# Linear attention's second pass: pairs of products joined to 104 columns, another order of products, and the prefix scan first

## The chip, the cores and the metric

The kernel runs on one NeuronCore of a Trainium2 chip. The metric is the time of one execution on the device in microseconds; the median of three runs is taken. The engines are named PE (TensorE), DVE (VectorE), ACT (ScalarE), POOL (GpSimd) and SP (the engine that only issues transfers here). All arithmetic that the change touches is in 32-bit floating point.

## The reference

Three stages follow each other. The change touches only the first, a linear attention with a state of 40 x 40 per head (4 batches, 8 heads, 768 positions):

```python
for t in range(S):
    y[:, :, t] = np.einsum('bhd,bhde->bhe', rt, state)
    Sa = np.einsum('bhde,bhe->bhd', state, at)
    state_decay = state * wt[:, :, None, :] - np.einsum('bhd,bhe->bhde', Sa, bt)
    state = state_decay + np.einsum('bhd,bhe->bhde', vt, kt)
```

The second stage routes each of 3,072 tokens to one of 8 experts by the largest of 8 logits (a product with `moe_w_gate`), two products with a ReLU between, weighted by the gate. The third is a dense layer with a leaky ReLU (320 to 2,048 to 320).

## The kernel before

Attention is done in chunks of 64 positions. There are 24 steps (`STEPS`): 12 chunks for each of two halves of the batch. A step handles 16 heads at once: two partition halves (rows 0 to 39 and 64 to 103 are live) times eight slots (`HS`). Every product of a step is 16 matmuls (`heads`: four slots times `COMBOS`, the four 64 x 64 quadrants of the array). The trace shows a 32-bit matmul as two records, so a group of 16 matmuls is 32 records and 32 weight loads.

The first pass (to 131 us) makes, per step, scans of the decay w over the chunk on DVE, products for the chunk's triangular system, and its inverse in blocks (POOL does most of the inverting, until about 294 us, beside the second pass). The scans are two: suffix products (`suffixes`, backward, into `suf`) and prefix products (`prefixes`, forward, into `wq`), the second started from the reciprocal of the first's end (`prefix_starts`).

The second pass (139 to 375 us) carries the state through the steps. PE runs one loop (`pe.Fori`, L930) with 18 groups, in this order by the names of the operands: alpha with the scaled state `swt` (and with `ax`, alpha brought across the halves by a transfer), values `vtm` with `g2`, the state turned (`eye,swt`), the keys turned (`eye,second`), u (`w_tm,inv`), m1 (`rr,vt`), `vtm,ktm`, the low part (`sa_tm,off`), `eye,st`, `m,ktm`, sa (`w_tm,inv`), sat (`inv,w_tm`), `rr,st`, `sa_tm,btm`, m2 (`rr,sat`), g2 (`alpha,second`), picks (`pick,yt`: rows of x and logits), `m,btm`. `arrive` is a wait on a semaphore. The products go to four pairs of PSUM banks (BA to BD). The new state is the sum of `vtm,ktm`, `eye,st` and `sa_tm,btm` in BD; the output is the sum of `m,ktm`, `rr,st` and `m,btm` in BB.

ACT copies products from PSUM to SBUF (L745 w_tm, L747 st, L749 ktm, L751 and L756 sa_tm, L758 sat, L738 picked) and spreads the inverse into `inv` (L722). DVE scales alpha (L454) and second (L451), masks m1, m2 and g2 (L482), adds the low part to w_tm (L529), scales the state (L548) and the output (L459), sums the gate parts (L464), and makes the scans for the step after next. The order on each engine is the order of the code; SP issues loads in the order of its own loop. After step 24 come the routing (from L561) and the experts.

Of the kernel before, what the change touches and what calls it, by code (L numbers as in the profile page):

```python
# [10 lines left out]
ALU = mybir.AluOpType  # L11
# [4 lines left out]
PARTS = 128  # L16
BATCH, HEADS, SEQ, DIM = 4, 8, 768, 40
HALF = PARTS // 2
C = 64
# [82 lines left out]
WIDE = C + 2  # L102
GROUP = PARTS // (4 * HS)
# [49 lines left out]
BLOCK_AT = B * B + B  # L153
BY_DVE, AT_DVE = 2, 11
# [5 lines left out]
def attention(nc, inp, dram, keep):  # L160

    with ExitStack() as ctx:
# [11 lines left out]
        alpha, second = (m_.sb(n, [PARTS, HS, C]) for n in ("alpha", "second"))  # L174
# [5 lines left out]
        btm, ktm, st = (m_.sb(n, [PARTS, HS, DIM]) for n in ("btm", "ktm", "st"))  # L180
        g2, m1, m2, sat, vt = (m_.sb(n, [PARTS, HS, C]) for n in ("g2", "m1", "m2", "sat", "vt"))
        rr = m_.sb("rr", [PARTS, HS + HP, C])
        vtm = m_.sb("vtm", [PARTS, HS + HP, DIM])
        inv = m_.sb("inv", [PARTS, HS, C])
        inv_in = ring("inv_in", 2, [PARTS, HS, B])
        w_tm, sa_tm, swt = (m_.sb(n, [PARTS, HS, DIM]) for n in ("w_tm", "sa_tm", "swt"))
# [4 lines left out]
        logit = m_.sb("logit", [PARTS, NTT, EXPERTS])  # L191
        ROUTE = NTT * EXPERTS
        late = m_.sb("late", [PARTS, 5 * ROUTE + NET * EXPERTS])

        def late_part(n, **sizes):
# [41 lines left out]
        s_set, s_suf, s_rw, s_wq, s_wc, s_second, s_alpha1, s_alpha0, s_alpha = (m_.sem(n) for n in (  # L237
            "s_set", "s_suf", "s_rw", "s_wq", "s_wc", "s_second", "s_alpha1", "s_alpha0", "s_alpha"))
        names = ("turned", "across", "joint", "g1", "bt", "w", "s", "u", "ktm", "z", "m1", "sa", "sat", "st", "g2", "m2", "y", "pick")
        did = {n: m_.sem("pe_" + n) for n in names}  # L240
        out_of = {n: m_.sem("ev_" + n) for n in names}
        s_settle = m_.sem("s_settle")
        s_xst = [m_.sem(f"s_xst{s}") for s in two]
        s_rows, s_iota = m_.sem("s_rows"), m_.sem("s_iota")
# [25 lines left out]
        def _(sp):  # L270
            def load_t(j):
                if j >= TR:
                    if j - TR < STEPS:
                        sp.wait_ge(s_alpha1, j - TR + 1)
                    elif j - TR == STEPS:
                        sp.wait_ge(s_alpha0, 1)
                    else:
                        sp.wait_ge(s_second, j - TR + 1)
                src = inp["wab"][j] if j < STEPS else inp["wak"][j - STEPS]
                sp.dma_start(t_in[j % TR][:, :], src).then_inc(s_t[j % TR], 16)  # L280
# [41 lines left out]
            def load_rr(k):  # L322
                if k >= 1:
                    sp.wait_ge(did["m2"], k)
                sp.dma_start(rr[:, :, :], inp["rr"][k]).then_inc(s_vt_rr, 16)

            def load_vtm(k):
                if k >= 1:
                    sp.wait_ge(did["z"], k)
                sp.dma_start(vtm[:, :, :], inp["vtm"][k]).then_inc(s_ax_vtm, 16)  # L330

            def load_vt(k):
                if k >= 1:
                    sp.wait_ge(did["m1"], k)
                sp.dma_start(vt[:, :, :], inp["vt"][k]).then_inc(s_vt_rr, 16)

            def cross_wq(k):
                sp.wait_ge(s_wc, k + 1)
                if k >= 3:
# [1255 lines left out]
```

## Time and profile before

| | |
|---|---|
| runs | 1055.56, 1056.46, 1059.53 us (median 1056.46) |
| profiled execution | 1057.93 us, its span 1056.2 us |
| PE, DVE, ACT, POOL busy over the span | 953.4, 710.1, 442.8, 269.8 us |
| first pass | 0 to 131 us, DVE busy 92% of its first 70 us |
| second pass | 139 to 375 us |
| routing and turn to the experts | 375 to 400 us |
| experts, dense layer | 400 to 678 us, 678 to 1056 us |

The span is cut into instructions by engine. "Idle before" is the time in which the engine had nothing running ahead of an instruction. A matmul's record includes the time in which its result drains, so records of one group overlap and the start of the next group tells more than the end of the last. A group's line gives the start of its first record, the time from there to the end of its last, and the number of records.

### The profile page before, as it was taken

To read this page: it belongs to the slowest core of one execution; us is meant where nothing else is said; L and a number is where in the kernel's file an instruction comes from. 1 tells how busy PE (TensorE), PEld (TensorE's weight loads), DVE (VectorE), ACT (ScalarE), POOL (GpSimd) and SP (SyncE) were. 2 spreads that over 40 slices of the span, in tenths; PEclk is the share of its full clock that TensorE was granted. 3 is DMA by queue.
4 is the path that set the end of the run, shared out by engine and by line. 5 is a ranking of instruction groups with operands and counts; after the bars stand their busy time and mean duration, and the time that the engine had idled before them with its cause. 6 is when DMAs were issued, how large, how long until landed. Compare 5 with 4: busy or idle time off the path is not lost. (4 is left out here: it accounts for less than half of the span.)

```text
span 1056.2 us, 48691 instructions
## 1 busy us (share of the span) xinstructions
PE 953.4 (90%) x21425; PEld 875.1 (83%) x21425; DVE 710.1 (67%) x1076; ACT 442.8 (42%) x940; POOL 269.8 (26%) x348
## 2 busy tenths in 40 slices
PE   3426779999999998999999999879999999999997
PEld 2426769999989958898999999668999999999997
DVE  8997947899988764554555555557665565656654
ACT  5525635755556604555555555513222212222211
POOL 1009989798910003213111100240001000000000
PEclk9999977999999999999999999989999999999999
DMA  7968856889888539999676755120100101010100
GB/s 234 256 192 212 216 142 202 254 270 262 259 251 255 171 119 296 310 297 303 192 246 213 228 169 168 42 77 10 39 4 26 25 1 25 2 26 1 25 1 26
DMA packets 118354, 159.62 MB, mean 151 GB/s; under 512 B 68516, under 2 KB 87860, under 8 KB 117908
## 3 DMA queue, kind: packets, MB, share of 16 engines
q1 hardware_dynamic: 103956, 125.12, 39.8%
q0 software_dynamic: 5872, 25.28, 8.0%
q10 hardware_dynamic: 8464, 8.43, 2.4%
q8 instruction: 36, 0.59, 0.2%
q14 instruction: 26, 0.21, 0.1%
HBM read 133.15 MB, written 19.23 MB: 144 GB/s over the span
## 5 line engine op out<-in xcount | busy, mean ns | idle before, releaser
L1466 ACT CAST g_hi<-g 128x512 fp32r<-128x512 f32 x96 | 59.5, 620 | 279.2 <-DVE g L1410 275.5
L1319 PE MATMUL y_bank<-w_out_hi,g_hi 128*128 128x320 f32 x380 | 119.1, 313 | 4.8 <-DVE g_lo L1384 2.9
L1107 PE MATMUL h_bank<-xt,w 128*128 128x128 f32 x992 | 121.4, 280 | 1.0 <-issue 0.8
L1147 DVE TENSOR_TENSOR w_lo<-w_all,w_hi 128x640 fp32r<-128x640 f32 x124 | 101.6, 825 | 29.1 <-ACT w_hi L1187 22.4
L1107 PEld LDWEIGHTS h_bank<-xt,w 128*128 128x128 f32 x992 | 114.5, 193 | 5.8 <-issue 1.9
L1319 PE MATMUL y_bank<-w_out_hi,g_lo 128*128 128x320 f32 x380 | 118.0, 311 | 0.0
L1319 PE MATMUL y_bank<-w_out_lo,g_hi 128*128 128x320 f32 x380 | 117.9, 310 | 0.0
L1406 DVE TENSOR_SCALAR neg<-h_bank,slope 128x512 f32<-128x512 f32 x96 | 71.9, 749 | 66.9 <-PE h_bank L1306 62.8
L1306 PE MATMUL h_bank<-xt_hi,w_in_hi 128*128 128x512 f32 x288 | 113.6, 394 | 0.5 <-DVE xt_hi L1367 0.5
L1306 PE MATMUL h_bank<-xt_hi,w_in_lo 128*128 128x512 f32 x288 | 112.7, 391 | 0.0
L1384 DVE TENSOR_TENSOR g_lo<-g,g_hi 128x512 fp32r<-128x512 f32 x96 | 66.5, 693 | 65.9 <-ACT g_hi L1466 63.8
L1140 DVE SCALAR_TENSOR_TENSOR ht_lo<-h_bank,ht_hi 128x512 fp32r<-128x512 f32 x62 | 42.7, 691 | 91.2 <-ACT ht_hi L1180 90.1
L1187 ACT CAST w_hi<-w_all 128x640 fp32r x124 | 89.8, 727 | 27.2 <-PE y_bank L1119 17.5
L127 POOL TENSOR_TENSOR solved<-solved,share 128x31 f32<-128x31 f32 (+15 forms) x124 | 96.6, 779 | 9.7
L782 PE MATMUL bank<-alpha,second 40*64 40x64 f32 x1568 | 45.2, 271 | 56.6 <-DVE alpha L454 55.8
L124 POOL TENSOR_TENSOR share<-solved,blk 128x31 f32<-128x31 f32 (+15 forms) x124 | 93.2, 752 | 9.7
L782 PEld LDWEIGHTS bank<-alpha,second 40*64 40x64 f32 x1568 | 39.1, 180 | 59.9 <-issue 59.9
L95 POOL DMA_INDIRECT x<-x_rows_mid,order x31 | 31.6, 1019 | 192.9 <-DVE order L607 96.7
L1319 PEld LDWEIGHTS y_bank<-w_out_hi,g_hi 128*128 128x128 f32 x380 | 71.9, 189 | 10.3 <-DVE g_lo L1384 4.0
L1119 PE MATMUL y_bank<-w_hi,ht_hi 128*128 128x320 f32 x248 | 79.1, 319 | 0.0
L1180 ACT ACTIVATE ht_hi<-h_bank 128x512 fp32r<-128x512 f32 x62 | 37.0, 598 | 100.0 <-PE h_bank L1107 95.3
L1119 PE MATMUL y_bank<-w_lo,ht_hi 128*128 128x320 f32 x248 | 76.7, 309 | 0.0
(213 smaller groups left out, 2146.3 us busy)
## 6 DMA issues: line engine op xcount, KB each, us to landing
w<-w_in SPq DMA_DIRECT2D x31, 1024.0 KB
t_in<-wab_in SPq DMA_DIRECT2D x24, 776.0 KB, 4.6
t_in<-wak_in SPq DMA_DIRECT2D x24, 776.0 KB, 6.0
w_all<-w_in POOLq DMA_DIRECT2D x8, 1280.0 KB, 9.4
rr<-rr_in SPq DMA_DIRECT2D x24, 384.0 KB, 3.4
w_rest<-w_in SPq DMA_DIRECT2D x62, 128.0 KB
vt<-vt_in SPq DMA_DIRECT2D x24, 256.0 KB, 3.8
vtm<-vtm_in SPq DMA_DIRECT2D x24, 240.0 KB, 3.4
```

Source lines behind the costliest of these rows:

```text
L124: link(eng.tensor_tensor(part, q[:, 0:j + 1, j:j + 1].to_broadcast(shape), h[:, j:j + 1, j + 1:B].to_broadcast(shape), ALU.mult))
L127: link(eng.tensor_tensor(rest, rest, part, ALU.subtract))
L782: last = pe.matmul(out[HALF * to:HALF * to + rows_out, row, n * i:n * i + n], lhs, rhs, start=opens and i == 0, stop=closes and i == HP - 1)
L1107: last = pe.matmul(h_bank[s][h][:, f * ET:(f + 1) * ET], w1[s][:, k, (FH * h + f) * PARTS:(FH * h + f + 1) * PARTS], xt[s][:, k, :], start ...
L1119: last = pe.matmul(y_bank[s][:, 0:FEAT], h[s][:, f, :], w[:, f, :], start=f == 0 and n == 0, stop=f == NF - 1 and n == 2)
L1147: dve.tensor_tensor(piece(w2_lo, p), of_expert(e, p), piece(w2_hi, p).bitcast(F32), ALU.subtract).then_inc(s_w2lo, 1)
L1187: act.copy(piece(w2_hi, p), of_expert(e, p)).then_inc(s_w2hi, 1)
L1306: last = pe.matmul(h_bank[j % 2][:, :], w[:, k, f * PARTS:(f + 1) * PARTS], x_part[b % 2][:, k, :], start=n == 0, stop=n == len(passes) - 1)
L1319: last = pe.matmul(y_bank[n][:, 0:FEAT], g_part[j % RING][:, n * PARTS:(n + 1) * PARTS], v[:, f, :], start=f == 0 and p == 0, stop=f == NF ...
L1384: dve.tensor_tensor(g_lo[j % RING][:, :], g[j % 2][:, :], g_hi[j % RING][:, :].bitcast(F32), ALU.subtract).then_inc(s_glo, 1)
L1406: dve.tensor_scalar(neg[j % 2][:, :], h_bank[j % 2][:, :], 0.0, keep.slope[:, f:f + 1], ALU.min, ALU.mult).then_inc(s_neg, 1)
L1466: act.copy(g_hi[j % RING][:, :], g[j % 2][:, :]).then_inc(s_ghi, 1)
```

## The change

In the second pass, four pairs of products with one stationary operand each are joined into products of 104 columns (`BOTH`). The moving operands stand side by side in new tiles: `alpha_eye` (alpha beside the identity), `eye_rr` (identity beside r), `v_m1` (values beside m1), `sa_m2` (sa beside m2). The state and the output now stand side by side in bank BD, so both are complete when the last group is. The loop of PE has 14 groups in another order. `vtm,g2` runs first, and alpha with the state waits for its end (`did["gv"]`), and for the scaled state. The keys are turned at the end of the step before, beside g2.

The prefix scan comes first in both passes and its end gives the decay of the chunk; the suffix scan starts from its reciprocal. The copy L448 falls away. The gate parts are copied by ACT (`gate_parts`) and reduced by DVE in two instructions at the end, not in one per step. ACT copies the values into `v_m1`. Loads of `t_in` (from the fourth on), `rr` and `vt` bring 112 partitions (`USED`) and not 128; `vtm` brings 8 slots and not 12. Some tiles lie on space of later stages.

```diff
+BOTH = C + DIM
+USED = HALF + 48
@@ DVE, the second pass
             for k in range(STEPS):
                 more = k + 1 < STEPS
-                if k >= 1:
-                    y_out(k - 1)
-                    if k >= 2:
-                        gates_of(k - 2)
-                    else:
-                        dve.sem_inc(out_of["pick"], 1)
                 dve.wait_ge(did["w"], k + 1)
                 if more:
-                    scaled_alpha(STEPS + k + 1, s_alpha)
+                    scaled_alpha(STEPS + k + 1).then_inc(s_alpha, 1)
                 if k + 2 < STEPS:
-                    suffixes(STEPS + k + 2)
-                dve.wait_ge(did["m1"], k + 1)
-                masked(m1, BB).then_inc(out_of["m1"], 1)
-                if k + 2 < STEPS:
-                    prefix_starts(STEPS + k + 2)
+                    if k >= 1:
+                        dve.wait_ge(out_of["y"], k + 1)
+                    prefixes(STEPS + k + 2)
+                    suffix_starts(STEPS + k + 2)
                 dve.wait_ge(did["z"], k + 1)
                 w_flat = w_tm[:, :, :].rearrange("q (r p) e -> q r (p e)", r=2)
                 dve.tensor_tensor(w_flat, w_flat, BA[:, :, 0:HP * DIM], ALU.add).then_inc(out_of["z"], 1)
+                dve.wait_ge(did["m1"], k + 1)
+                masked(m1, wide(BB)).then_inc(out_of["m1"], 1)
                 if more:
-                    dve.wait_ge(did["ktm"], k + 1)
                     scaled_second(STEPS + k + 1)
                 else:
                     dve.sem_inc(s_second, 1)
                 if k + 2 < STEPS:
-                    prefixes(STEPS + k + 2)
+                    suffixes(STEPS + k + 2)
                 elif k + 2 == STEPS:
                     dve.wait_ge(s_iota, 8)
+                    dve.wait_ge(s_gates, NTT - LATE)
+                    first_choices(gates_of(FIRST))
                     choices_top(FIRST, first_choices)
...
@@ ACT
+            def key_out(k):
+                act.wait_ge(out_of["g2"], k + 1)
+                if k >= 1:
+                    act.wait_ge(did["st"], k)
+                act.copy(by_row(ktm[:, :, :]), BC[:, :, 0:HP * BOTH].rearrange("q r (p t) -> q r p t", t=BOTH)[:, :, :, C:BOTH]).then_inc(out_of["ktm"], 1)
...
+                act.copy(v_m1[:, :, 0:DIM], vtm[:, :, :]).then_inc(s_beside, 1)
...
@@ PE, the loop of the second pass
             with pe.Fori(1, STEPS + 1) as i:
                 arrive(s_ax_vtm, 48 * i)
+                arrive(out_of["g2"], i)
+                heads(g2_v, BA, DIM, closes=False, done="gv")
                 arrive(out_of["st"], i)
-                heads(alpha_s, BA, DIM, closes=False)
-                arrive(out_of["g2"], i)
-                heads(g2_v, BA, DIM, opens=False, done="w")
+                arrive(did["gv"], i)
+                heads(alpha_s, BA, DIM, opens=False, done="w")
+                heads(turned_state, BB, DIM, done="s")
+                arrive(out_of["w"], i)
+                arrive(out_of["ktm"], i)
+                heads(u_product, BC, DIM, done="u")
                 arrive(out_of["y"], i)
...
```

PE, the loop of the second pass, before. A row is an instruction or a run of equal ones; the last numbers are stationary by moving columns, and the tiles are named by what they hold (`m` is m1 or m2).

```order
L782 MATMUL bank<-vtm,g 64x40 [waits ev_g2]
L782 MATMUL bank<-vtm,g 64x40 x15
L782 MATMUL bank<-eye,swt 40x40 [waits ev_y]
L782 MATMUL bank<-eye,swt 40x40 x15
L782 MATMUL bank<-eye,second 64x40 [waits ev_pick]
L782 MATMUL bank<-eye,second 64x40 x15
L782 MATMUL bank<-w_tm,inv 64x40 [waits ev_w]
L782 MATMUL bank<-w_tm,inv 64x40 x15
```

The same place after the change: the tail of alpha with the state, and u behind it.

```order
L793 MATMUL bank<-vtm,g 64x40 [waits s_ax_vtm,ev_g2]
L793 MATMUL bank<-vtm,g 64x40 x15
L793 MATMUL bank<-swt,alpha_eye 64x40 [waits ev_st,pe_gv]
...
L793 MATMUL bank<-eye,swt 40x40 x16
L793 MATMUL bank<-w_tm,inv 64x40 [waits ev_w,ev_ktm]
L793 MATMUL bank<-w_tm,inv 64x40 x15
```

`vtm,g` has moved ahead of the state's products and is waited for; the turned keys no longer stand ahead of u.

PE, the end of the loop, before: from sat to the jump.

```order
L782 MATMUL bank<-inv,w_tm 40x64 x16
L782 MATMUL bank<-rr,st 40x64 x16
L782 MATMUL bank<-sa_tm,btm 40x40 [waits ev_sa]
L782 MATMUL bank<-sa_tm,btm 40x40 x15
L782 MATMUL bank<-rr,sat 64x64 [waits ev_sat]
L782 MATMUL bank<-rr,sat 64x64 x15
L772 REGISTER_ALU
L782 MATMUL bank<-alpha,second 64x64 [waits s_second]
L782 MATMUL bank<-alpha,second 64x64 x15
L772 REGISTER_ALU
L844 MATMUL bank<-pick,yt 64x48 [waits ev_st]
```

The same place after (`w_0` holds sat, `x_1` holds btm, `v_m` and `sa_m` are `v_m1` and `sa_m2`).

```order
L793 MATMUL bank<-eye_rr,st 40x104 [waits s_rows]
L793 MATMUL bank<-eye_rr,st 40x104 x15
L793 MATMUL bank<-eye_rr,w_0 64x64 [waits ev_sat]
L793 MATMUL bank<-eye_rr,w_0 64x64 x15
L782 REGISTER_ALU
L793 MATMUL bank<-alpha_eye,second 64x104 [waits s_second,ev_sa]
L793 MATMUL bank<-alpha_eye,second 64x104 x15
L793 MATMUL bank<-v_m,ktm 40x104 [waits ev_m1,s_beside]
L793 MATMUL bank<-v_m,ktm 40x104 x15
L793 MATMUL bank<-sa_m,x_1 40x104 [waits ev_m2,s_btm]
L793 MATMUL bank<-sa_m,x_1 40x104 x15
```

The product that completes the state was followed by four groups (m2, g2, picks, `m,btm`); now it is the last group of the loop.

DVE, one step of the second pass, before (`TENSOR_TENSOR_SCAN` is printed as SCALAR_TENSOR_TENSOR).

```order
L454 TENSOR_TENSOR alpha<-t_in,wq 128x512 [waits pe_w]
L435 SCALAR_TENSOR_TENSOR suf<-t_in,restart 128x528 [waits s_second,s_t2]
L482 TENSOR_TENSOR m<-bank,later 128x512 [waits pe_m1]
L440 RECIPROCAL restart<-suf 128x8 [waits s_suf]
L529 TENSOR_TENSOR w_tm<-w_tm,bank 128x320 [waits pe_z]
L451 TENSOR_TENSOR second<-t_in,suf 128x512 [waits pe_ktm]
L444 SCALAR_TENSOR_TENSOR wq<-t_in,restart 128x528 [waits s_rw]
L448 COPY wq<-suf 128x8 [waits s_wq]
L548 TENSOR_TENSOR swt<-bank,wq 128x320 [waits s_wqx1,pe_st]
L482 TENSOR_TENSOR m<-bank,later 128x512 [waits pe_m2]
L482 TENSOR_TENSOR g<-bank,later 128x512 [waits pe_g2]
L459 TENSOR_TENSOR yt<-bank,wq 128x512 [waits s_wqx0,pe_y]
```

The same step after.

```order
L469 TENSOR_TENSOR alpha_eye<-t_in,wq 128x8x64 [waits pe_w]
L450 SCALAR_TENSOR_TENSOR wq<-t_in,restart 128x528 [waits s_suf,s_t0,ev_y]
L455 RECIPROCAL restart<-wq 128x8 [waits s_wq]
L530 TENSOR_TENSOR w_tm<-w_tm,bank 128x320 [waits pe_z]
L490 TENSOR_TENSOR v_m<-bank,later 128x8x64 [waits pe_m1]
L466 TENSOR_TENSOR second<-t_in,suf 128x512 [waits s_suf]
L461 SCALAR_TENSOR_TENSOR suf<-t_in,restart 128x528 [waits s_second,s_rw]
L490 TENSOR_TENSOR sa_m<-bank,later 128x8x64 [waits pe_m2]
L490 TENSOR_TENSOR g<-bank,later 128x512 [waits pe_g2]
L557 TENSOR_TENSOR swt<-bank,wq 128x320 [waits s_wqx1,pe_st]
```

The mask of m1 and the add of z have changed places, a whole scan stands ahead of the add, another ahead of the mask of m2, and the scaled state comes after both masks.

## Rows read from the trace of the kernel before

**Rows 1.** Windows of the second pass: start and end, length, busy by engine, clock, DMA.

```profile
138.00:160.00 22.00, 16.40 (x704) 15.74 (x708) 9.32 (x14) 6.93 (x18) 19.14 (x38) 0.67 0.52 147
160.00:370.00 210.00, 201.54 (x12819) 192.46 (x12815) 178.24 (x285) 125.57 (x313) 118.49 (x162) 0.98 0.82 239
```

**Rows 2.** Timeline, one step without GpSimd: start, length, engine, line, operation, tiles.

```profile
329.57 0.22 PE L782 MATMUL bank<-swt,alpha 40*64 40x40 f32 x1 [0.24 <-issue]
330.03 0.68 PE L782 MATMUL bank<-vtm,g 64*64 64x40 f32 x32
330.77 0.43 ACT L745 COPY w_tm<-bank 128x320 f32<-128x320 f32 x1 [1.54 <-PE bank L782]
331.34 0.68 PE L782 MATMUL bank<-w_tm,inv 64*64 64x40 f32 x32
332.84 0.67 PE L782 MATMUL bank<-sa_tm,off 32*64 32x40 f32 x32
333.44 0.52 PE L782 MATMUL bank<-eye,st 40*40 40x40 f32 x32
333.58 0.49 DVE L529 TENSOR_TENSOR w_tm<-w_tm,bank 128x320 f32<-128x320 f32 x1
333.77 0.64 PE L782 MATMUL bank<-m,ktm 64*40 64x64 f32 x32
334.23 0.66 PE L782 MATMUL bank<-w_tm,inv 64*64 64x40 f32 x32
334.67 0.67 PE L782 MATMUL bank<-inv,w_tm 64*40 64x64 f32 x32
335.40 0.59 ACT L758 COPY sat<-bank 128x512 f32<-128x512 f32 x1
336.13 0.69 PE L782 MATMUL bank<-rr,sat 40*64 40x64 f32 x32
336.62 0.68 PE L782 MATMUL bank<-alpha,second 40*64 40x64 f32 x32
336.88 0.69 DVE L482 TENSOR_TENSOR m<-bank,later 128x512 f32<-128x512 f32 x1 [0.24 <-PE bank L782]
337.72 0.66 PE L782 MATMUL bank<-m,btm 64*40 64x64 f32 x32
338.61 0.22 PE L782 MATMUL bank<-swt,alpha 40*64 40x40 f32 x1 [0.23 <-issue]
```

**Rows 3.** Timeline, output scaling of two steps, fourteen steps apart.

```profile
170.68 0.69 DVE L459 TENSOR_TENSOR yt<-bank,wq 128x512 f32<-128x512 f32 x1 [0.21 <-PE bank L782]
300.85 0.69 DVE L459 TENSOR_TENSOR yt<-bank,wq 128x512 f32<-128x512 f32 x1 [0.27 <-PE bank L782]
```

**Rows 4.** Timeline, filler matmuls of 512 columns after the second pass.

```profile
378.82 6.68 PE L849 MATMUL bank<-t_in,ones 128*128 128x512 f32 x15
```

**Rows 5.** Timeline, the scaling of the state at step 22.

```profile
363.63 0.49 DVE L548 TENSOR_TENSOR swt<-bank,wq 128x320 f32<-128x320 f32 x1 [0.34 <-PE bank L782]
```

**Rows 6.** Timeline, PE at the loop's turn while the clock is low.

```profile
155.83 1.10 PE L782 MATMUL bank<-m,btm 64*40 64x64 f32 x32
156.92 0.29 PE L782 MATMUL bank<-swt,alpha 40*64 40x40 f32 x1
```

**Rows 7.** Timeline, reductions on DVE in step 22 and in the routing.

```profile
362.01 0.32 DVE L471 TENSOR_REDUCE top<-logit 128x21 f32<-128x168 f32 x1
377.19 0.18 DVE L471 TENSOR_REDUCE top<-logit 128x3 f32<-128x24 f32 x1
383.17 0.61 DVE L595 TENSOR_REDUCE total<-late 128x24 f32<-128x192 f32 x1
```

**Rows 8.** Timeline, DVE, suffix scans of two steps of the first pass.

```profile
37.69 1.25 DVE L435 TENSOR_TENSOR_SCAN suf<-t_in,restart 128x528 f32<-128x528 f32 x1
41.71 1.25 DVE L435 TENSOR_TENSOR_SCAN suf<-t_in,restart 128x528 f32<-128x528 f32 x1
```

**Rows 9.** Timeline, PE in the first turn of the second pass's loop.

```profile
145.56 0.36 PE L782 MATMUL bank<-vtm,ktm 64*40 64x40 f32 x5 [3.32 <-issue]
```

More of the change, by code:

```diff
@@ L173, in attention @@
         wq = [t[:, 0:HS, :] for t in wq_both]
-        alpha, second = (m_.sb(n, [PARTS, HS, C]) for n in ("alpha", "second"))
+        second = m_.sb("second", [PARTS, HS, C])
+        alpha_eye = m_.sb("alpha_eye", [PARTS, HS, BOTH])
+        alpha = alpha_eye[:, :, 0:C]
         ax = m_.sb("ax", [PARTS, HP, C])
@@ L542, in _ @@
                     choices_one(FIRST, first_choices).then_inc(s_hot, 1)
+                dve.wait_ge(did["m2"], k + 1)
+                masked(m2, wide(BA)).then_inc(out_of["m2"], 1)
+                if more:
+                    dve.wait_ge(did["g2"], k + 2)
+                    masked(g2[:, :, :], beside(BC, 0, C)).then_inc(out_of["g2"], 1)
                 dve.wait_ge(did["st"], k + 1)
+                dve.wait_ge(s_wqx[k % 2], 32 * turn(k))
                 if (k + 1) % NCHUNK == 0:
@@ L742, in _ @@
             prepare(0)
+            key_out(0)
             for k in range(STEPS):
@@ L776, in eye, with heads @@
                 return keep.eye[live(h), HALF * h:HALF * h + DIM]
-            def heads(product, out, n, opens=True, closes=True, done=None):
+            def heads(product, out, n, opens=True, closes=True, done=None, first=0, step=None):
                 for i in range(HP):
+                    at = first + (step or n) * i
                     for q, m in COMBOS:
                         row, to, rows_out, lhs, rhs = product(i, q, m)
-                        last = pe.matmul(out[HALF * to:HALF * to + rows_out, row, n * i:n * i + n], lhs, rhs,
+                        last = pe.matmul(out[HALF * to:HALF * to + rows_out, row, at:at + n], lhs, rhs,
                                          start=opens and i == 0, stop=closes and i == HP - 1)
@@ L819, in g2_v @@
             def g2_v(i, q, m):
-                return q, q ^ m, C, g2[rows(q), slot(q ^ m, i), :], vtm[rows(q), slot(m, i), :]
+                return q, q ^ m, C, g2[rows(m), slot(q ^ m, i), :], vtm[rows(m), slot(q, i), :]
             def m1_product(i, q, m):
@@ L899, in bt_product @@
                 heads(turned(second), BB, DIM, done="bt")
-            for n in ("g1", "bt", "y", "pick", "turned", "across", "joint"):
+            for n in ("g1", "bt", "y", "turned", "across", "joint"):
                 pe.sem_inc(out_of[n], 1)
+            pe.sem_inc(s_rows, 1)
             with pe.Fori(1, AT_JOIN + 1) as i:
```

206 lines of the change are left out of this document (98 added, 108 removed).

## The prediction

> **What bounds the kernel now.** I read the windows first. The second pass of attention, which holds all that matters of the change, runs from 139 us to about 375 us. In the 210 us from 160 on, TensorE is busy for 201.5 and VectorE for 178.2 [rows 1]. That looks like a full TensorE. The timeline of one step says otherwise. Matmuls are pipelined, so a group counts as busy for some 0.2 us after its last start. I therefore read starts, not busy times. One step goes from 329.57 to 338.61, 9.04 us [rows 2]. Its PE groups are either spaced by streaming alone (0.44 to 0.49 for 64 columns or 64 stationary columns, 0.33 for 40 by 40) or held by a round trip through another engine. The round trips, start of a group to start of the group that reads it, are:
>
> - through ScalarE, w: vtm,g starts 330.03, its end is 0.68 later, the copy starts 330.77 and takes 0.43, u starts 331.34. That is 1.31.
> - through VectorE, z: 332.84 to 333.58, 0.49 of add, sa at 334.23. That is 1.39.
> - through ScalarE for sat, behind the copy of sa: 334.23 to 335.40, 0.59, m2 at 336.13. That is 1.90, and PE waits there.
> - the mask of m2: 336.13 to 336.88, 0.69, the last group at 337.72. That is 1.59, and PE waits there too.
> - the turn of the loop: last group 337.72, first of the next step 338.61. That is 0.89, of which 0.45 is streaming and 0.44 is nothing but the jump.
>
> So the step is 0.46 (alpha) + 1.31 + 1.50 (u to low) + 1.39 + 1.90 + 1.59 + 0.89 = 9.04. It is a chain of latencies that PE fills well. Eighteen groups leave little of it empty. While GpSimd runs beside VectorE a step is a little longer: 14 steps from 170.68 to 300.85 are 9.30 each [rows 3].
>
> **The change part by part.** *Joined pairs.* Eight groups become four of 104 columns. The price of 104 is not in the trace. A 64-column group is .44 and a 40-column one .33, whose slope gives 0.62. The 512-column matmuls, 15 records in 6.68, are 0.445 each with the drain of the last [rows 4], and eight records to each quadrant that is 8 x 0.445 x 104/512 = 0.72. I take 0.71, since at half clock (below) time goes with the columns. A pair of 40 and 64 now costs 0.77, so three pairs gain 0.06 each and the fourth (key turn with g2, both near 0.47) about 0.22: 0.4 us of streaming a step. The columns stay the same; only the fixed part goes.
>
> *The other order.* The fourteen groups must now cover the same round trips. Going round the new step:
>
> - alpha,swt now comes after vtm,g and is what ends w. Start of alpha to start of u: the same 1.31. Only the turned state (0.33) lies under it, not key turn as well: alpha 0.46 + 0.33 = 0.79, so PE stands 0.5.
> - u to the low part: the same kind of ScalarE round trip, 1.31. Between them stand only the picks (0.9 in all), so it is 1.31 where it was 1.50.
> - low part to sa: 1.39, as before, with m1 alone under it.
> - sa to m2: 1.90, as before (from_s, 104 wide, lies under it).
> - m2 to the last group: g2 with key turn, then keys, so 0.49 + 0.71 + 0.71 = 1.91 where it was 1.59. The mask of m2 is now covered.
> - last group to the next alpha. Before 0.89. Now the state comes out of the *last* group. Over VectorE: end at 0.71 + 0.24, 0.06 to start, 0.49 of scaling [rows 5], 0.15 back: 1.64. Over PE: the jump, then vtm,g, whose *end* alpha now waits for (a new wait on PE's own semaphore): jump, 0.68, 0.15. In a cold turn, where the last group streams for 0.83, the turn is 155.83 to 156.92, 1.09 [rows 6], so only 0.26 of the jump shows behind a longer group. Then vtm,g starts at 0.97 and alpha at 1.80. I take 1.80. Its bounds are 1.64 and 1.99 (the full 0.44).
>
> Sum: 1.31 + 1.31 + 1.39 + 1.90 + 1.91 + 1.80 = 9.62, against 9.04: +0.58 a step. The low bound takes 0.62 for the joined price in three places on the path and no semaphore time: 9.2. The high one takes 1.99 and 0.1 for double waits: 9.9.
>
> The Trainium skill bears on the jump: its page "TensorE: Matmul & The Clock Gate" (opening table) gives TensorE a queue 64 deep. A group here is 64 records, so by that rule the whole jump would lie under a 0.71 group and the state's 1.64 would decide; the sum would be some 3.5 us lower over the pass. The trace agrees in direction only (0.44 shrinks to 0.26 and not to nothing).
>
> VectorE: the prefix scan (1.3, 1.7 beside GpSimd) now stands ahead of the add of z. Alpha 1.0 + scan 1.7 + reciprocal 0.2 make z about 0.25 late in the steps with GpSimd. Before, these steps lose 0.26 as well [rows 3], so I add nothing. The gate reduction and the copy of the decay leave VectorE; nobody waited for them. ScalarE's new copies (values, gate parts) stand before u's copy or after it, where ScalarE was idle. The key copy waits for the last group and ends 0.5 us after it, before w's copy is due.
>
> 22 steps at full clock x 0.58 = +12.8 (bounds +4 and +19).
>
> *The first two steps.* They run at the lower level, 1.2 GHz (0.67 granted over 138 to 160) [rows 1]; from 156.92 the second takes 13.8 [rows 3, 6]. There PE streams without a gap. New: nine wide groups x 0.84, two narrow 0.3, four of 1.40 is 13.8, and waits of about 1 (alpha on vtm,g's end, u, the jump) are added. With the first step partly standing anyway: +1.6 for both (0 to 2.5).
>
> *Step 22.* All gate sums of 21 tiles are now one reduction, 1,344 elements, put before the choices and thus before the mask of m2. Reductions: 24 elements 0.18, 168 in 0.32 (slope 1.0 ns), strided 192 in 0.61 [rows 7]. So 1.5 to 3.9 us. The choices take 1.28 (362.01 to 0.34 before 363.63). VectorE has about 1.8 to spare there, as the scans are gone. Late by 1.0 to 3.4: +2.2.
>
> *The tail.* The output scaling now follows the memset of the state (0.3), the last gates come 0.2 sooner: +0.3 (-0.3 to 0.6).
>
> *First pass.* Same five VectorE instructions a step, in a new order; each reads the result of one before as now, and 4.02 from scan to scan [rows 8] stays. PE's g1 waits for the last of them as before. 112 partitions instead of 128 and the smaller values load spare DMA time that nobody waited for. Both at nothing; what hides the loads is that they are issued a step or more ahead, and if that failed in the new order I would see waits on rr or vtm.
>
> Sum: 12.8 + 1.6 + 2.2 + 0.3 = +16.9 on the execution's own 1057.9 (span 1056.2), so 1074.8. The median of the runs shown is 1.5 lower, 1056.5, so I forecast 1074 (rounded up). Bounds: +4 gives 1061, +26 gives 1082.
>
> **Rivals.** *PE is the bound, as its busy share says.* Then the gain of streaming counts and the new exposures lie under PE's queue: 22 x (-0.4 - 0.18 for the m2 wait) = -12.8, plus 2.2 for step 22: 1046. For it: 201.5 of 210 busy, and VectorE near full in places. Against: starts show PE standing for round trips, and the new order takes cover from three of them. It decides if alpha to u comes out under 1.0. Chance 0.14.
>
> *The clock.* The low stretch began when PE had stood for 3.3 us in the first turn of the loop [rows 9]. With fewer records to bring in, the stand may be short enough that the clock stays at 2.4 GHz, or it comes back a step sooner: up to -9 (two steps of 13.8 to 18 where 9.6 and the stalls would do), so 1065. The Trainium skill ("TensorE: Matmul & The Clock Gate", Part 1) has activity releasing the clock; what gaps of half a microsecond do to it no row here shows. Chance 0.14.
> *The clock the other way:* the new cold steps have gaps (0.5 + 0.3 + 0.3) where the old ones had none, and the higher level may come later. Each further step at 1.2 GHz costs 5: 1079 to 1089. Chance 0.10.
>
> *The change adds exposures and saves as much* (joined price 0.62, jump hidden, fast reduction, a start at full clock): about 1056. Chance 0.06.
>
> **How the numbers follow.** Forecast 0.56, its own range 1061 to 1082. Less than 0.5% (5 us) is what a measurement of this kernel can tell from no change. Faster 0.14 (first rival), same 0.06, slower 0.80. The range 1056 to 1086 leaves out the first rival and the worst of the clock.
>
> **What would show it.** Right: PE groups of 104 columns 0.7 apart; a step of 9.6; PE idle about 0.5 before w_tm,inv, 0.4 before the low part, and a stand before alpha of 0.8 after the last group's streaming. A late m2 mask at step 22, 2 us. The first pass to 131 us unchanged. Wrong: steps under 9.1, or joined groups under 0.6 apart.

## The result, and the profile after

The changed kernel ran in 1119.88 us (median of four runs: 1108.38, 1114.09, 1125.67, 1132.31); the kernel before in 1056.37 (four runs, 1055.56 to 1059.53). The ratio is 1.0517, interval 1.0458 to 1.0576, and counts only the two faster runs (mean granted clock 0.941 and 0.935), as the two slower ones ran at 0.919 and 0.912. It is slower, as forecast, but by 55 us by the ratio (63 by the median of all four) and not by 17, and the time lies above the range.

The profiled execution took 1108.38 us, its span is 1106.6, that is 50.4 more than before. Its page: engines with busy time, then PE's busy tenths and the granted clock in 40 slices, then the transfers.

```profile
PE 995.1 (90%) x18353; PEld 911.7 (82%) x18353; DVE 708.7 (64%) x1034; ACT 454.2 (41%) x988; POOL 264.3 (24%) x348
PE   3536898998889899899999999988999999999997
PEclk9999999668986968899999999999999999999999
DMA packets 155649, 151.20 MB, mean 137 GB/s; under 512 B 113060, under 2 KB 129332, under 8 KB 155204
```

TensorE is busy 42 us longer than before (953.4) though its columns are the same. The clock line says why: in the slices of the second pass (139 to 427 us) it drops again and again. Before, it was low only at the pass's start [rows 1].

The first and the last scaling of the output give the length of the pass, as [rows 3] did for 14 steps of it. Timeline of after, DVE:

```profile
154.45 0.68 DVE L560 TENSOR_TENSOR yt<-bank,wq 128x512 f32<-128x512 f32 x1
427.12 0.63 DVE L560 TENSOR_TENSOR yt<-bank,wq 128x512 f32<-128x512 f32 x1
```

Read at each of the 24 scalings, the 23 steps between take:

| | steps in us, start of one output scaling to the next |
|---|---|
| before | 13.7, then 22 steps of 9.0 to 9.8, mean 9.28 |
| after | 10.2 9.8 10.5 9.8 13.9 13.8 13.9 13.8 13.8 9.8 10.5 9.9 10.0 10.5 13.8 13.9 13.8 9.8 10.2 9.9 13.7 13.8 13.7 |

There are two kinds of step: 12 of about 10.1 and 11 of 13.8. Take the ordinary one first, to compare with [rows 2]. Timeline of after, PE, one step at the higher clock (start, length, tiles):

```profile
175.46 0.22 PE L793 MATMUL bank<-swt,alpha_eye 40*64 40x40 f32 x1 [0.17 <-PE bank L793]
176.92 0.68 PE L793 MATMUL bank<-w_tm,inv 64*64 64x40 f32 x32 [0.48 <-ACT w_tm L756]
178.23 0.67 PE L793 MATMUL bank<-sa_m,off 32*64 32x40 f32 x32 [0.17 <-ACT sa_m L761]
179.60 0.68 PE L793 MATMUL bank<-w_tm,inv 64*64 64x40 f32 x32
181.51 0.69 PE L793 MATMUL bank<-eye_rr,w 40*64 40x64 f32 x32
182.03 0.94 PE L793 MATMUL bank<-alpha_eye,second 40*64 40x104 f32 x32
182.76 0.92 PE L793 MATMUL bank<-v_m,ktm 64*40 64x104 f32 x32
183.59 0.92 PE L793 MATMUL bank<-sa_m,x 64*40 64x104 f32 x32
184.56 0.68 PE L793 MATMUL bank<-vtm,g 64*64 64x40 f32 x32
185.41 0.22 PE L793 MATMUL bank<-swt,alpha_eye 40*64 40x40 f32 x1 [0.17 <-PE bank L793]
```

| from start to start | forecast | measured |
|---|---|---|
| alpha to u | 1.31 | 1.46 |
| u to the low part | 1.31 | 1.31 |
| low part to sa | 1.39 | 1.37 |
| sa to m2 | 1.90 | 1.91 |
| m2 to the last group (`sa_m,x`) | 1.91 | 2.08 |
| last group to the next alpha | 1.80 | 1.82 |
| the step | 9.62 | 9.95 |

The chain was foreseen nearly right, stands included: 0.48 before u, 0.17 more before the low part (0.4 was forecast), 0.97 + 0.85 round the turn. Joined groups start 0.73 apart, one 0.83.

Now a step of 13.8. The timeline of after, PE, from the ordinary part of a step into the long one and out of it:

```profile
196.86 0.68 PE L793 MATMUL bank<-w_tm,inv 64*64 64x40 f32 x32 [0.48 <-ACT w_tm L756]
197.32 0.69 PE L858 MATMUL bank<-pick,yt 40*64 40x48 f32 x32
198.17 0.94 PE L793 MATMUL bank<-sa_m,off 32*64 32x40 f32 x32 [0.17 <-ACT sa_m L761]
199.05 1.13 PE L793 MATMUL bank<-eye_rr,w 40*64 40x64 f32 x32
206.63 1.61 PE L793 MATMUL bank<-sa_m,x 64*40 64x104 f32 x32
208.02 0.91 PE L793 MATMUL bank<-vtm,g 64*64 64x40 f32 x32
210.57 0.68 PE L793 MATMUL bank<-w_tm,inv 64*64 64x40 f32 x32 [0.48 <-ACT w_tm L756]
211.03 0.69 PE L858 MATMUL bank<-pick,yt 40*64 40x48 f32 x32
211.88 0.99 PE L793 MATMUL bank<-sa_m,off 32*64 32x40 f32 x32 [0.17 <-ACT sa_m L761]
```

The group u takes 0.68; at the low part, records stretch (0.94, then 1.13 where 0.69 is usual), joined groups take 1.61 and start 1.39 apart; at `vtm,g` they shrink again. The next u, at 210.57, is as quick as the one at 196.86; at the low part the clock goes once more. The windows of after say the same (start:end, length, busy PE and PEld, DVE, ACT, POOL, then the clock, DMA share, GB/s):

```profile
160.00:200.00 40.00, 35.20 (x1743) 31.74 (x1735) 31.95 (x43) 27.72 (x76) 35.95 (x53) 0.98 0.92 205
200.00:206.00 6.00, 6.00 (x188) 6.00 (x184) 4.35 (x5) 4.36 (x12) 5.38 (x8) 0.50 0.68 148
208.00:210.00 2.00, 1.81 (x104) 1.70 (x96) 1.24 (x3) 0.58 (x2) 1.76 (x4) 0.84 0.02 8
210.00:212.00 2.00, 1.36 (x84) 1.20 (x74) 2.00 (x2) 1.73 (x6) 1.84 (x3) 1.00 0.57 112
212.00:214.00 2.00, 2.00 (x76) 1.92 (x79) 1.23 (x3) 0.31 (x1) 1.84 (x3) 0.51 0.83 265
214.00:222.00 8.00, 8.00 (x233) 8.00 (x229) 4.79 (x5) 4.36 (x12) 7.29 (x10) 0.50 0.81 189
```

So a long step is one fall of the clock to 1.2 GHz. It begins a moment after the stands before u and the low part, and some 10 us of gapless work follow at half speed (198.4 to 208.6). Then the clock comes back and the next stands follow. All eleven falls begin in this place, between the start of the picks behind u and 0.4 us into the low part. Ten microseconds at half speed do 5 us of work, yet a fall costs only 3.8 us: the slower groups fill up the stands that are there anyway. Ahead of the series TensorE was less full than before the change: busy for 35.2 us of the 40 from 160 us on, where before it was 201.5 of 210 [rows 1].

**Where the 50.4 us are.** Steps 2 to 23 of each trace: 22 x 9.28 = 204.2 before; after, 11 of 10.05 and 11 of 13.8, 262.4 in all. At 10.05 each they would be 221.1.

| | forecast | profiled |
|---|---|---|
| 22 steps, the new chain | +12.8 | +16.9 |
| 11 falls of the clock | 0 | +41.3 |
| start to the first output scaling, and the first step (13.7 to 10.2) | +1.6 | -2.5 - 3.5 |
| step 22, late mask | +2.2 | inside a long step |
| after the last scaling (681.3 to 679.5) | +0.3 | -1.8 |
| sum | +16.9 | +50.4 |

The waits of PE in after, 139 to 420 us (total, times, longest), show the stands by their cause:

```profile
PE bank L793 <- ACT w_tm L756: 11.3, 24, 0.5
PE bank L793 <- PE bank L793: 3.9, 20, 0.3
PE bank L793 <- ACT sa_m L761: 3.6, 22, 0.2
PE bank L793 <- DMA ax<-alpha_eye: 1.9, 4, 0.6
```

### The profile page after: what moved, and what is told of

Same layout as the page of the kernel before. It is cut to its first block and busy times, and to the rows that moved or that the text cites. A ratio compares the mean times of both kernels' runs of the same rounds, so it can differ in the third digit from the quotient of the medians.

```text
span 1106.6 us, 42604 instructions
## 1 busy us (share of the span) xinstructions
PE 995.1 (90%) x18353; PEld 911.7 (82%) x18353; DVE 708.7 (64%) x1034; ACT 454.2 (41%) x988; POOL 264.3 (24%) x348
## 5 line engine op out<-in xcount | busy, mean ns | idle before, releaser
L793 PE MATMUL bank<-alpha_eye,second 40*64 40x104 f32 (+1 forms) x1568 | 59.6, 318 | 55.1 <-DVE second L466 54.2
L793 PEld LDWEIGHTS bank<-alpha_eye,second 40*64 40x64 f32 x1568 | 50.8, 199 | 58.3 <-issue 58.3
L125 POOL TENSOR_TENSOR share<-solved,blk 128x31 f32<-128x31 f32 (+15 forms) x124 | 87.7, 707 | 9.7
```

What stands on the lines that cost most here:

```text
L125: link(eng.tensor_tensor(part, q[:, 0:j + 1, j:j + 1].to_broadcast(shape), h[:, j:j + 1, j + 1:B].to_broadcast(shape), ALU.mult))
L793: last = pe.matmul(out[HALF * to:HALF * to + rows_out, row, at:at + n], lhs, rhs, start=opens and i == 0, stop=closes and i == HP - 1)
```

## The experiments

The first theory: the stands of the new order bring the clock down; work put into them should hold it, and remove the steps of 13.8. Its rivals: the joined matmuls themselves bring it down; or the order costs what it costs, and the clock is no part of it. A filler below is a group of matmuls into columns that nobody reads. A stand is a time in which TensorE had nothing to run, and a fall is a stretch in which the granted clock is at 1.2 GHz. Ratios are to the kernel before on the same chip. The mean clock, and every count of falls or waits below, is that of the one profiled execution of each kernel; the other executions differ somewhat.

| | median us | ratio | interval | mean clock, profiled |
|---|---|---|---|---|
| e1_fill_u | 1084.37 | 1.0317 | 1.0257 to 1.0376 | 0.984 |
| e2_fill_all | 1075.92 | 1.0249 | 1.0176 to 1.0322 | 0.987 |
| e3_split | 1117.05 | 1.0591 | 1.0519 to 1.0662 | 0.939 |
| e4_b_gap | 1063.69 | 1.0085 | 1.0046 to 1.0125 | 0.978 |
| e5_fill_rr_ax | 1080.61 | 1.0243 | 1.0189 to 1.0297 | 0.975 |
| e6_fill_ax | 1074.23 | 1.0210 | 1.0151 to 1.0270 | 0.986 |
| e7_fill_split | 1095.61 | 1.0429 | 1.0365 to 1.0492 | 0.986 |
| e8_b_cold | 1055.75 | 1.0020 | 0.9989 to 1.0051 | 0.983 |
| e9_b_gaps | 1084.09 | 1.0245 | 1.0185 to 1.0305 | 0.979 |
| e10_fill_gl | 1083.43 | 1.0234 | 1.0177 to 1.0290 | 0.971 |
| e11_unjoin_alpha | 1079.00 | 1.0211 | 1.0152 to 1.0271 | 0.983 |
| e12_fill_128 | 1080.26 | 1.0234 | 1.0176 to 1.0293 | 0.979 |

### One filler ahead of u (e1_fill_u)

```diff
-                arrive(out_of["w"], i)
                 arrive(out_of["ktm"], i)
+                heads(turned_state, BC, DIM, first=HP * C)
+                arrive(out_of["w"], i)
                 heads(u_product, BC, DIM, done="u")
```

> The changed kernel with one more group of 16 matmuls (the turned state once more, into columns nobody reads) in the gap ahead of u, 0.33 us of work where PE stands 0.48 a step. Theory G (gaps let the clock fall): the chain is as long as before, about 9.9 a step at 2.4 GHz, but fewer or no stretches at 1.2 GHz, so 1062 to 1100. Rival D (the clock falls for another reason, such as the dense 104-column groups): more work only, no fewer low stretches, 1110 to 1130.

1084.37 us, a ratio of 1.0317 where after has 1.0517, and the intervals do not touch. Extra work made the kernel faster, by 28 us between the two profiled executions (spans 1106.6 and 1078.8). Only one fall is left in the steps from 157 to 396 us (a step of 12.8), and it begins 2.3 us behind a stand of 0.86 for alpha's crossing; the other 22 take 9.6 to 11.1, but for one of 12.0 at the end. The edit also puts the wait for the keys ahead of the wait for w; what that alone is worth is seen in e10. The other three runs of e1 have mean clocks of 0.971 to 0.976, so they had more low time than the profiled one.

### Fillers in all three stands (e2_fill_all)

```diff
                 heads(g2_v, BA, DIM, closes=False, done="gv")
+                heads(from_e, BB, DIM, first=HP * C)
...
+                heads(turned_state, BA, DIM, first=HP * C)
```

These are behind `vtm,g2` and ahead of the low part, beside e1's.

> The same filler in three gaps: behind vtm,g (ahead of alpha), ahead of u, ahead of the low part. Theory G: the whole pass at 2.4 GHz, steps of 9.8 to 10, about 1062 (1108 less 12 low steps of 3.85). Rival D: no fewer low stretches, 1110 or more.

1075.92 us. No fall is left from 155 us until step 22, at 383 us. Window of e2 (columns as above):

```profile
160.00:360.00 200.00, 188.20 (x10526) 173.91 (x10525) 155.00 (x214) 119.95 (x315) 113.84 (x163) 1.00 0.90 208
```

The ratio is 1.0249, with three more groups a step. By the two profiled executions it is 32.1 us less than after (spans 1106.6 and 1074.5), and that adds up: the falls give back 41.3; the crossing of alpha, waited for 8.9 us instead of 1.9, takes 7.0, and the late mask 2.1. These two are also why the 1062 that was expected was missed. What is left over before is mostly the chain: the steps are 9.9 where nothing is late, against 9.28. Its step 22 shows the late mask on its own. Timeline of e2, PE:

```profile
380.94 0.92 PE L793 MATMUL bank<-v_m,ktm 64*40 64x104 f32 x32
383.95 1.63 PE L793 MATMUL bank<-sa_m,x 64*40 64x104 f32 x32 [2.09 <-DVE sa_m L490]
```

PE stands 2.09 us for the mask, and the clock is low when it goes on (1.63 for the group), so that step takes 12.9. In after the reduction that makes it late took 2.60 us. Timeline of after, DVE:

```profile
406.15 2.60 DVE L472 TENSOR_REDUCE logit<-w 128x168 f32<-128x1344 f32 x1
410.12 0.69 DVE L490 TENSOR_TENSOR sa_m<-bank,later 128x512 f32<-128x512 f32 x1
```

### The joined matmuls taken apart (e3_split)

The order stays; each product of 104 columns becomes one of 64 and one of 40.

```diff
-                        last = pe.matmul(out[HALF * to:HALF * to + rows_out, row, at:at + n], lhs, rhs,
-                                         start=opens and i == 0, stop=closes and i == HP - 1)
+                        for part in (slice(0, C), slice(C, n)) if n == BOTH else (slice(0, n),):
+                            last = pe.matmul(out[HALF * to:HALF * to + rows_out, row, at + part.start:at + part.stop], lhs, rhs[:, part], ...
```

> The changed kernel in its new order, with each joined product of 104 columns done as two matmuls of 64 and 40, as before the change. It is some 0.35 us a step more streaming, on the path in three places (+0.1 to +0.3 a step at full clock). If the gaps of the new order alone bring the clock down (theory G), it falls here as well, time 1105 to 1135. If joining brings it down (rival D), the clock stays up: steps of 10.2 and about 1065 to 1070.

1117.05 us, ratio 1.0591, clock 0.939: at least as slow as after, and the clock falls as often, 13 times from 160 us on, for 3.6 to 14 us. The joining is not what brings it down. Most falls begin around the same part of the step (u, the picks, the low part), four of them 1.0 to 1.7 us behind the low part's stand. Timeline of e3, PE, the start of one:

```profile
202.58 0.99 PE L794 MATMUL bank<-w_tm,inv 64*64 64x40 f32 x32 [0.51 <-ACT w_tm L756]
```

### The kernel before with one stand (e4_b_gap)

```diff
-                heads(turned(second), BD, DIM, done="ktm")
                 arrive(out_of["w"], i)
+                heads(turned(second), BD, DIM, done="ktm")
```

> The kernel before with only the wait for w_tm moved ahead of the turned keys, so that PE stands about 0.5 us a step there; no joined products. Chain: at most 9.04 + 0.5 a step, so +11 us if the clock holds, 1068. Theory G: the gap alone makes the clock fall in places as it does in the changed kernel, 1080 to 1115. Rival D: 1066 to 1070.

1063.69 us (10 runs; the kernel before 1054.62 in 13). The steps become 9.5 to 10.0, mean 9.62 for 9.28, and the clock shows no fall in the steady pass. The stand is 0.32 us by the trace (23 times, 7.4 us) and not the 0.5 that was planned. It costs its place in the chain and nothing more: 22 steps by 0.33. By the expectation this is the rival's outcome: one such stand does not bring the clock down.

### Crossing of alpha earlier, rr loaded in longer pieces (e5_fill_rr_ax, e6_fill_ax)

In e2, PE waits 11 times for the transfer of alpha across the halves, 8.9 us in all. In after this transfer lands 5.3 us after its issue, where before took 3.3. One row of the DMA issues in each, before and after (KB each, median us to landing):

```profile
ax<-alpha ACTq DMA_DIRECT2D x46, 64.0 KB, 3.3
```

```profile
ax<-alpha_eye ACTq DMA_DIRECT2D x46, 64.0 KB, 5.3
```

The new tiles hold alpha and r in rows of 104 columns, of which 64 are moved, so the 1 KB that the crossing moves in each partition goes as pieces of 256 bytes: the packets of the pass rise from 47,752 to 83,693. e6 is e2 with the crossing issued ahead of the rows of x; e5 also loads r with the identity beside it, in one piece.

```diff
-                if k >= 1:
-                    rows_of(k - 1)
                 cross_alpha(k + 1)
+                if k >= 1:
+                    rows_of(k - 1)
```

```diff
-                sp.dma_start(rr[0:USED], inp["rr"][k][0:USED]).then_inc(s_vt_rr, 16)
+                sp.dma_start(eye_rr[0:USED], inp["rr"][k][0:USED]).then_inc(s_vt_rr, 16)
```

> The kernel with the three fillers, and only alpha's crossing issued before the copies of the picked rows (0.65 us sooner). If the late issue alone is to blame, the whole gain: about 1067. If the small packets are, a part: 0.65 of each of 11 waits, 1070 to 1074.

> The kernel with the three fillers, and two edits on transfers: the identity beside r comes in with r from memory, so that a partition of eye_rr is one piece and not twelve of 256 bytes, and alpha's crossing is issued before the copies of the picked rows. With the clock held, every second step of the filler kernel is about 1 us longer, and PE waits 8.9 us in all for ax. Theory T (the new layouts make small packets, and ax lands late): these waits go, steps of 9.8 to 9.9, about 9 us less than the filler kernel (1076): 1065 to 1068. Rival: the long steps come from DVE beside GpSimd, no gain, 1074 to 1077.

e6: 1074.23 us, waits for the crossing 7 times, 5.1 us. e5: 1080.61, 8 times, 10.0 us, although its packets from 139 to 400 us are 55,187. Longer pieces but more bytes (r 546 KB a step for 336) made the crossing no earlier. So the earlier issue is worth some 4 us of waits, and e5 does not separate number of packets from bytes. e5 also had two falls, in steps of 16.4 and 17.3, behind stands of 1.48 and 2.14 us for this transfer. In e6 PE stood as long as the first of them without a fall. Timeline of e6, and the window behind it:

```profile
349.43 0.68 PE L793 MATMUL bank<-vtm,g 64*64 64x40 f32 x32 [1.51 <-DMA ax<-alpha_eye]
```

```profile
350.00:360.00 10.00, 9.80 (x575) 9.08 (x570) 7.08 (x11) 5.80 (x15) 0.00 (x0) 1.00 0.87 194
```

### Fillers, and the pairs apart (e7_fill_split)

The edits of e2 and e3 together.

> The kernel with the three fillers and the joined products done as 64 and 40 columns again. With the clock held it shows what joining gives by itself: on the path g2 with keys, values and m1, and the last group, each some 0.05 to 0.2 shorter joined. Forecast by group starts: +0.3 to +0.4 a step, 7 to 10 us more than the filler kernel, 1083 to 1086. Rival: joining gives nothing, 1076.

1095.61 us, against 1083 to 1086 expected. All steps are at 10.7 to 11.0 but the one with the late mask (12.6), and no fall is left from 162 us to the end of the pass. Against e2 this prices the joining with the clock out of the way. A step is 0.9 longer than e2's where nothing is late there (9.9). The mean step is only 0.42 longer (10.88 for 10.46), as e7 never waits for the crossing, which lengthens e2's steps. The profiled executions differ by 15 us, the ratios by 0.018, some 19 us. Timeline of e7, PE, for the joined groups' rows above:

```profile
329.81 1.19 PE L794 MATMUL bank<-alpha_eye,second 40*64 40x64 f32 x64
330.81 1.02 PE L794 MATMUL bank<-v_m,ktm 64*40 64x64 f32 x64
331.73 1.02 PE L794 MATMUL bank<-sa_m,x 64*40 64x64 f32 x64
333.15 0.68 PE L794 MATMUL bank<-vtm,g 64*64 64x40 f32 x32 [0.40 <-issue]
```

Pairs issued alternately, 64 then 40 columns, start 1.00 and 0.92 apart instead of 0.73, and the turn of the loop shows 0.40 of issue behind them. They are dearer than the two separate groups of before (0.46 + 0.33), so not all of the 0.9 is to the credit of joining.

### The kernel before, entering the pass differently (e8_b_cold)

The filler matmuls ahead of the pass left out:

```diff
-            warm(2)
...
-            warm(3)
```

> The kernel before without the five filler matmuls ahead of the second pass, so that it enters the loop at 1.2 GHz. In the kernel before, PE enters at 2.4 GHz, stands 3.3 us in the first turn and then runs two steps at 1.2 GHz (18.0 and 13.8). The changed kernel entered at 1.2 GHz, had no such stand, and only its first step was slow (15.8). Theory: the same here, about 6 us less, 1048 to 1051. Rival: the clock stays low for two or more steps as before, 1056 to 1065.

1055.75 us, the same as before (ratio 1.0020), and not the 1048 to 1051 expected. Entering the loop at the lower clock, as after does, is therefore not what gives after its better start. TensorE stood for 1.10 and 1.84 us in the first turn, and the clock was back for good at 167 us, 2 us sooner than before; no later fall in the steady pass. (That e8 and after enter at the lower clock is read from their groups, 1.1 us each; the clock column reads 1.00 there until 153 us in e8.)

### The kernel before with three stands (e9_b_gaps)

The last test of the theory, from the other side: if stands alone bring the clock down, three waits moved one group ahead should do to before what the change did.

```diff
-                heads(turned(second), BD, DIM, done="ktm")
                 arrive(out_of["w"], i)
+                heads(turned(second), BD, DIM, done="ktm")
...
-                heads(from_k(lambda i, q, m: at_m(vtm, i, q, m, rows(m))), BD, DIM, closes=False)
                 arrive(out_of["u"], i)
+                heads(from_k(lambda i, q, m: at_m(vtm, i, q, m, rows(m))), BD, DIM, closes=False)
...
+                arrive(out_of["z"], i)
                 heads(from_s(lambda i, q, m: eye(m)), BD, DIM, opens=False, closes=False)
                 arrive(out_of["m1"], i)
                 heads(from_k(lambda i, q, m: m1[rows(m), slot(q, i), :]), BB, C, closes=False)
-                arrive(out_of["z"], i)
                 heads(sa_product, BC, DIM, done="sa")
```

> The kernel before with three waits moved one group ahead and nothing else: for w_tm ahead of the turned keys, for u ahead of values by keys, for z ahead of the turned state; PE stands about 1.5 us more a step, its work is unchanged. If gaps alone bring the clock down, the kernel before must do it too: steps alternate between 10.5 at 2.4 GHz and about 14 at 1.2 GHz, 1100 to 1130. If the fall needs something else of the change, the clock holds and it is 22 x 1.5 more: 1085 to 1090.

1084.09 us. That is just under the range of the case "the clock holds" (1085 to 1090) and far from the 1100 to 1130 that was expected if stands alone bring the clock down: as it was put, the theory failed this test. By the trace PE stands 0.32 ahead of the turned keys and 0.70 ahead of the turned state in each step; the third wait moved hardly shows. The steps are 10.5 (chain longer by 1.2: 22 steps, 26 us), and two are 11.8 and 11.9. The two are falls. Timeline of e9, PE, through the first of them:

```profile
240.11 0.65 PE L782 MATMUL bank<-eye,st 40*40 40x40 f32 x30 [0.70 <-DVE w_tm L529]
241.35 1.10 PE L782 MATMUL bank<-w_tm,inv 64*64 64x40 f32 x32
242.17 1.14 PE L782 MATMUL bank<-inv,w_tm 64*40 64x64 f32 x32
243.80 0.51 PE L782 MATMUL bank<-sa_tm,btm 64*40 64x40 f32 x32
244.13 0.69 PE L782 MATMUL bank<-rr,sat 40*64 40x64 f32 x32
```

It begins right behind the stand of 0.70 and ends within 4 us, at a cost of 1.3; the other, at 336 us, does the same. So two falls come into the old order with the stands, with no joined group in it. But they are two and short, where after has eleven and long, and the fullness is the same. Window of e9:

```profile
180.00:360.00 180.00, 158.37 (x9752) 147.94 (x9756) 141.20 (x221) 95.73 (x241) 94.57 (x140) 0.98 0.79 227
```

88% busy, as in after's 35.2 of 40 (0.98) just before its series begins. The busy share by itself does not tell how often the clock falls.

### Fillers in two stands of three (e10_fill_gl)

As e2, without the one ahead of u.

> The changed kernel with fillers behind vtm,g and ahead of the low part only; the gap ahead of u stays open (0.5 us). If the sum of the gaps decides, two fillers do as much as the first run's single one or more: few low stretches, 1076 to 1088. If the gap ahead of u is the one that matters, low stretches stay: 1095 to 1115.

1083.43 us. Two falls in the pass, steps of 16.7 and 16.5, and one at the end behind the late mask. The two come behind stands of 1.75 and 1.58 us for the crossing of alpha. Timeline of e10, PE:

```profile
166.70 0.68 PE L793 MATMUL bank<-vtm,g 64*64 64x40 f32 x32 [1.75 <-DMA ax<-alpha_eye]
182.52 0.22 PE L793 MATMUL bank<-swt,alpha_eye 40*64 40x40 f32 x1
183.82 0.68 PE L793 MATMUL bank<-w_tm,inv 64*64 64x40 f32 x32 [0.32 <-ACT w_tm L756]
```

So no one of the stands is the cause: filling only u's (e1) leaves one fall, filling only the two others leaves two. The series of after is gone in both, and the falls that remain before step 22 in e1, e5, e10 and e12 all come within 2.4 us of a stand of 0.86 us or more for the crossing.

The last two lines show something else. Alpha to u is 1.30 to 1.33 here in 23 of 24 steps, and 1.45 to 1.51 in every step of after behind the first. This kernel waits for the keys first, which are there already, and then for w; after waits for w and then for the keys. The stand ahead of u is therefore 0.32 here and 0.48 in after. The other order of two waits would give after 0.16 a step, some 3.5 us.

### Alpha in a tile of its own (e11_unjoin_alpha), 128 partitions (e12_fill_128)

Both start from e6. e11 gives alpha its own tile and makes g2 and the key turn two groups again; e12 sets `USED = PARTS`.

```diff
-        alpha_eye = m_.sb("alpha_eye", [PARTS, HS, BOTH])
-        alpha = alpha_eye[:, :, 0:C]
+        alpha = m_.sb("alpha", [PARTS, HS, C])[:, :, :]
...
+            def g2_and_keys(done):
+                heads(g2_alone, BC, C, closes=False, step=BOTH)
+                heads(turned(second), BC, DIM, opens=False, first=C, step=BOTH, done=done)
```

> Three fillers, early crossing, and alpha in a tile of its own again: g2 and the turned keys are two groups, the crossing's pieces are 1024 bytes and not 256. PE's waits for ax (5.1 us in the kernel it stands beside) go if packets are their cause: 22 x 0.27 for the pair less 5 for the waits, about equal, 1073 to 1077. If the waits stay, packets are not their cause: 1078 to 1082.

> Three fillers, early crossing, and all loads with 128 partitions again (14% more bytes on t_in, rr, vt). If the transfer engines are what makes ax late, the waits grow from 5 to 8 or 10 us: 1077 to 1080. If 112 partitions save nothing that is waited for: 1074, no difference.

e11: 1079.00 us. Waits for the crossing go from 5.1 us to 0.6, and the step is 10.1 for 9.9: the pair joined was worth 0.2 a step (forecast 0.22), and its tile cost as much in late transfers (mean step 10.30 in both, ratio 1.0211 and 1.0210). So it is the crossing's own small pieces that make it late. e12: 1080.26, its interval overlaps e6's; waits for the crossing as in e6 (7 times, 5.1 us), ordinary steps 9.9 to 10.8, one fall that e6 lacks (7 us long, behind a stand of 0.88 for the crossing) and a longer one at step 22. The waits were expected to grow to 8 or 10 us if the bytes were what counts; they did not, so the 112 partitions change nothing that shows.

## Why the prediction was wrong, point by point

- **The step that failed is "22 steps at full clock x 0.58".** The chain (0.58) was nearly right; "at full clock" was not. The prediction worked out stands of 0.5, 0.3 and 0.3 for TensorE and did not ask what the clock would do in the steady pass. Eleven falls cost 41.3 of the 50.4 us. Shown by e1 and e2: extra matmuls in the stands, with nothing else changed but the order of two waits (3.5 us, e10), take 28 and 32 us away in the profiled executions. Shown not to be the joining: e3 falls as after does, e9 falls without any joined group.
- **The rival "the clock the other way"** (0.10) had the right mechanism and the wrong place: it let the gaps prolong the cold start by a step or two, 1079 to 1089. The start was in fact better, and the falls came later, from 198 us on, in a pass that had been at full clock for 40 us. The sentence that no row shows what gaps of half a microsecond do was true, and the range should have been opened for it. The Trainium skill speaks of it ("TensorE: Matmul & The Clock Gate", section "A second HAM failure mode: psum-queue depth-cycling"): in a kernel whose TensorE idles briefly between groups, the clock goes up and down. The trace agrees, with eleven falls behind stands of 0.48 and 0.17 us; in the old order one stand of 0.32 a step brought none (e4). By that sentence the rival would have deserved a larger chance and a price for each fall.
- **The step.** Forecast 9.62, measured 9.95 in the row-by-row step: 0.15 of the 0.33 at u, where PE waits for w and then for the keys (e10, with the two waits the other way round, has 1.30), 0.17 between m2 and the last group. The 0.17 belongs to this step, where the mask of m2 came behind a slow scan on VectorE; in the next one that stretch is 1.97 and the turn 1.97. The upper bound had 0.1 for double waits. Over 22 steps +16.9 for +12.8, inside its bounds of 4 and 19. e6, with the clock held, measures 1074.23 us, next to the forecast; but there terms cancel (a better start against late crossings), so only its step of 9.9 bears the chain out.
- **Joined groups:** 0.73 apart for 0.71, and 1.39 at the lower clock for 1.40. The fourth pair 0.2 for 0.22 (e11). Right.
- **The turn of the loop:** 1.82 for 1.80, made of the end of `vtm,g` and not of the state's scaling. Right; it is 1.78 to 1.97 in the ordinary steps where no transfer or scaling is late, inside the bounds of 1.64 and 1.99, so the jump is not hidden.
- **The start:** forecast +1.6, measured -6.0. The first pass is unchanged, as forecast: the second pass's first product starts at 138.8 us for 138.9. The rival of a clock that comes back sooner (0.14, -9) was nearer. The first turn shows no stand like the 3.32 us of [rows 9] (its longest is 0.34) and the clock is up by the second step. Whether the one brings the other was not separated: e8 has shorter stands in the first turn too and gains nothing.
- **Step 22:** reduction 2.60 us (bounds 1.5 to 3.9), PE late by 2.09 in e2 (forecast 2.2); in after the lower clock hides it. Right. That it can also bring a fall was missed.
- **Loads at nothing:** 112 partitions yes (e12). The new stride no: the crossing of alpha lands 2 us later, PE waits for it 4 times in after (1.9 us), 11 times (8.9) where the falls no longer cover it. The prediction counted the bytes and not the pieces; with alpha in its own tile the waits are 0.6 us (e11).
- **"PE is the bound, 1046":** excluded. More work on PE made the kernel faster.

**What stays open.** In the new order the stands are what lets the clock fall: with work in them the falls go. They are not enough by themselves, as the old order with stands of 0.32 and 0.70 us shows. What else it takes, which stand does it, and for how long the clock stays low, no quantity here tells. e9 and after are equally full and differ by two falls to eleven; falls last 4 us in e9, 10 in after, 14 in e5 and e10. A stand of 1.51 us brought none in e6, one of 1.48 did in e5. In after a fall ends where the next stands wait, which may be why they come in series; that was only argued. Whether PE's own wait for the end of `vtm,g` could be spared wasn't tried, since the product that follows adds to the same bank.

## What to carry to other kernels

Count the time in which TensorE stands, even by halves of a microsecond, as a risk of its own: a change that puts short waits into a TensorE that was full may pay in clock a multiple of the waits, or nothing (e4). A few matmuls that nobody reads, put into the stands, tell in one run how much of a slowdown is the clock. And when operands are put side by side to join products, look at what else reads those tiles: a transfer of part of each row falls into small pieces.

## What the runs showed of the hardware

- The clock fell in the middle of a pass that had been at 2.4 GHz for 40 us, with no stand over 0.5 us in the 20 us ahead of it (after, 198 us). Every fall of the steady pass in after, e1, e3, e5, e9, e10 and e12 began within 2.4 us of a stand; where stands are as close as in after, that alone proves little. In after TensorE then worked without a gap at 1.2 GHz for some 10 us before it was back.
- A fall cost 3.8 us where about 10 us passed at half speed (after), and 1.3 us for 4 (e9).
- Matmuls of 64 and 40 columns issued alternately with one stationary operand: 0.92 to 1.00 for 64 records (e7), joined 0.73 (after).
- The same 64 KB across the halves: 3.3 us to landing in pieces of 1 KB (before), 5.3 in pieces of 256 bytes (after), beside other transfers that differ too.
- Of two waits in a row ahead of a group on TensorE, the one that is long satisfied costs 0.16 us when it comes last and nothing when it comes first: alpha to u 1.46 in after, 1.30 in e10.
